# A routed expert stage with its slot table read in one load, a later first split of w_in, and gate steps placed ahead of the w2 splits

## The reference

```python
attn_out = _attn_ref(x, state)                 # two cross reads: x (8,8,512,64), state (8,8,32,64)
x = attn_out.transpose(0, 2, 1, 3).reshape(B * S, H * D)     # 4352 rows of 512

# routed experts: E = 8, F = 1024
logits = xn @ en.T / tau                       # xn, en: rows divided by their norm
expert_idx = np.argmax(logits, axis=1)
gate_w = softmax(logits)[expert_idx]
for e in range(E):
    h = np.maximum(x[mask] @ w1[e], 0.0)
    out[mask] = gate_w[mask, None] * (h @ w2[e])

# dense block: d_ff = 2048
r = np.maximum(x @ w_in, 0.0)
return (s * (r * r) + b) @ w_out
```

## Time and profile before

| | us |
|---|---|
| median of 3 runs | 1513.04 (1512.64 to 1514.85) |
| profiled execution | 1512.6 |
| its span, first to last instruction | 1510.9 |
| PE busy | 1361.9 (90%) |
| DVE busy | 656.1 (43%) |
| ACT busy | 510.0 (34%) |
| POOL busy | 146.9 (10%) |

### The profile page before, as it was taken

The page is one execution under the profiler, slowest core; times in us unless marked ns, Lnnn a source line. Parts: engine busy times, 40 slices in busy tenths (PEclk is TensorE's granted clock), DMA queues, the critical chain, the costliest instruction groups (busy, mean ns, idle before and its releaser), DMA issues.

```text
span 1510.9 us, 22781 instructions
## 1 busy us (share of the span) xinstructions
PE 1361.9 (90%) x6875; PEld 1123.5 (74%) x6876; DVE 656.1 (43%) x1646; ACT 510.0 (34%) x977; POOL 146.9 (10%) x186
## 2 busy tenths in 40 slices
PE   5887224999999999999899999999999999999995
PEld 4655213787888888887788888888888888888884
DVE  4766512456656456555652232323223232322322
ACT  3655202345545345444332222222222222222221
POOL 1222210001111001101400010100001010000101
PEclk9988556999999999999899999999999999999998
DMA  8752212434434124314100010100101010010000
GB/s 214 144 122 64 63 16 51 151 110 162 159 115 168 43 104 164 111 43 168 42 15 29 1 56 0 56 0 14 42 0 56 0 56 0 0 56 0 28 0 28
DMA packets 81043, 100.07 MB, mean 66 GB/s; under 512 B 50152, under 2 KB 50408, under 8 KB 79984
## 3 DMA queue, kind: packets, MB, share of 16 engines
q1 hardware_dynamic: 68336, 69.59, 15.7%
q0 software_dynamic: 7200, 20.08, 4.1%
q10 hardware_dynamic: 5472, 9.96, 1.7%
HBM read 71.11 MB, written 28.64 MB: 66 GB/s over the span
## 4 chain that ended last, share of the span: by engine, by line
PE 79%; DVE 5%; issue 4%; ACT 3%; SPq 3%; DMA 2%; ACTq 2%; POOL 1%; DVEq 0%; another core or an unknown queue 0%; POOLq 0%
PE bank_a L1343 25%; PE bank_n L1362 13%; PE bank_t L1362 12%; PE bank_a L1277 10%; PE bank_n L1302 10%; DVE w_lo L963 1%; PE bank_t L1288 1%; PE bank_t L1112 1%; SPq L337 1%; SPq L384 1%; DMA x_tok<-st_rows 1%; PE bank_a L1095 1%; PE bank_n L1264 1%; ACT x_rows L555 1%; PE bank_a L1183 1%
## 5 line engine op out<-in xcount | busy, mean ns | idle before, releaser
L1047 DVE TENSOR_TENSOR sq<-rel 128x512 f32<-128x512 f32 (+1 forms) x144 | 95.5, 663 | 484.6 <-ACT rel L710 484.6
L710 ACT ACTIVATE rel<-bank_a 128x512 f32<-128x512 f32 (+1 forms) x144 | 82.8, 575 | 548.1 <-PE bank_a L1343 548.1
L1343 PE MATMUL bank_a<-y_hi,w_in_hi 128*128 128x512 f32 (+1 forms) x576 | 218.9, 380 | 4.6 <-DVE y_lo L1039 4.5
L1343 PE MATMUL bank_a<-y_hi,w_in_lo 128*128 128x512 f32 (+1 forms) x576 | 218.4, 379 | 0.0
L1343 PE MATMUL bank_a<-y_lo,w_in_hi 128*128 128x512 f32 (+1 forms) x576 | 218.3, 379 | 0.0
L1343 PEld LDWEIGHTS bank_a<-y_hi,w_in_hi 128*128 128x128 f32 x576 | 109.4, 190 | 26.2 <-DVE y_lo L1039 5.0
L1343 PEld LDWEIGHTS bank_a<-y_lo,w_in_hi 128*128 128x128 f32 x576 | 109.4, 190 | 20.6 <-issue 0.2
L1343 PEld LDWEIGHTS bank_a<-y_hi,w_in_lo 128*128 128x128 f32 x576 | 109.4, 190 | 20.1
L1302 PE MATMUL bank_n<-w_hi,hid_hi 128*128 128x512 f32 x304 | 119.1, 392 | 4.2 <-DVE hid_lo L970 4.2
L1302 PE MATMUL bank_n<-w_lo,hid_hi 128*128 128x512 f32 x304 | 119.0, 391 | 0.0
L1302 PE MATMUL bank_n<-w_hi,hid_lo 128*128 128x512 f32 x304 | 119.0, 391 | 0.0
(11 more groups left out here) (198 smaller groups left out, 2082.1 us busy)
## 6 DMA issues: line engine op xcount, KB each, us to landing
w_raw<-in_moe_w SPq DMA_DIRECT2D x16, 2048.0 KB, 9.7
moe_tok<-yg ACTq DMA_DIRECT2D x38, 256.0 KB, 2.0
x_tok<-x_rows SPq DMA_DIRECT2D x8, 1088.0 KB, 5.7
x_m<-in_x SPq DMA_DIRECT2D x8, 1024.0 KB
y_rows<-moe_tok SPq DMA_DIRECT2D x8, 1024.0 KB, 5.1
win_raw<-in_moe_w_in SPq DMA_DIRECT2D x8, 512.0 KB, 9.7
w_raw<-in_moe_w_out SPq DMA_DIRECT2D x1, 4096.0 KB, 15.1
idx_all<-slot_tab SPq DMA_DIRECT2D x43, 0.5 KB, 2.0
```

Source lines behind the costliest of these rows:

```text
L710: nc.scalar.activation(rel[:, k, 0:cols], ps_g[k][:, 0:cols], ACT.Relu).then_inc(rel_ready, 1)
L1047: nc.vector.tensor_tensor(sq[:, 0:cols], rel[:, k, 0:cols], rel[:, k, 0:cols], ALU.mult).then_inc(sq_ready, 1)
L1343: last = nc.tensor.matmul(ps_g[n % 2][:, 0:cols], w[:, wc], a[:, c, 0:cols], start=(c == 0 and w is w_in_hi and a is y_hi), stop=(c == DC ...
```

## The change

The slot table is now f32 and has room for TCAP·128 = 4608 entries per expert, 36 tiles' worth. SP reads all of it in one DMA into `slot_sb` (96 partitions, 3 pieces of 128 words); PE turns the three pieces into one PSUM bank, and DVE casts them into `idx_all`, which now has a column for every possible tile (288). A tile's column number is `slots_of`, read by POOL before each copy. SP's loads of w_in chunk 0 and of expert 1's weights follow the first gather directly, and the eight copies to `moe_id` (now f32) come after them. The ids for the scatter are loaded as f32 and cast by POOL. On ACT and DVE the split of w_in chunk 0 moves behind the hidden split of tile 0. In DVE's loop the gate steps of tile g+3 move ahead of the w2 splits.

```diff
+    TCAP = (NTOK + P - 1) // P + 2
+    TQ = E * TCAP // 3
-    CAP = NTOK
-    ZCOLS = (E * CAP + 8 * P) // P
+    CAP = TCAP * P
+    ZCOLS = E * CAP // P
...
+        slot_sb = sb(am, "slot_sb", [TQ, 3, P], f32)
+        sb(am, "hole", [P, 1408], f32)
+        idx_all = sb(am, "idx_all", [P, E * TCAP], i32)
...
-            def load_idx(g, done):
-                src = slot_tab[0:P, :] if g == 0 else slot_tab[ds(slots_of(sp, g), P), :]
-                sp.dma_start(idx_all[:, g:g + 1], src).then_inc(done, 16)
+            def copy_ids():
+                for e in range(E):
...
             sp.wait_ge(slots_written, 16 * (TPB + 1) * B)
-            with nc.allow_non_contiguous_dma(reason="one word per row"):
-                load_idx(0, idx_first)
-                sp.wait_ge(tab_ready, 1)
-                for g in range(1, NEAR):
-                    load_idx(g, idx_next)
-                sp.wait_ge(gathered, 16)
-                for g in range(NEAR, NSLOT):
-                    load_idx(g, idx_loaded)
+            sp.dma_start(slot_sb[:], slot_tab.rearrange("(k t q) o -> t k (q o)", k=3, q=P)).then_inc(slot_loaded, 16)
+            sp.wait_ge(tab_ready, 1)
+            sp.wait_ge(gathered, 16)
             load_win(0)
-            for e in range(E):
...
             for e in range(1, E):
                 sp.wait_ge(w1_ready, WS * e)
                 sp.dma_start(w_raw[:, 0:WCOLS], w1[e].rearrange("(c p) n -> p c n", p=P)).then_inc(w1_loaded, 16)
...
                 load_win(e)
                 sp.wait_ge(w2_ready, WS * e)
                 sp.dma_start(w_raw[:, WCOLS:2 * WCOLS], w2[e].rearrange("(c p) n -> p c n", p=P)).then_inc(w2_loaded, 16)
+                if e == 1:
+                    copy_ids()
...
-                nc.gpsimd.tensor_copy(g_idx[:], idx_all[:, ds(g, 1)]).then_inc(idx_turn, 1)
+                nc.gpsimd.tensor_copy(g_idx[:], idx_all[:, ds(0 if starts(g) else slots_of(pool, g), 1)]).then_inc(idx_turn, 1)
...
             def scatter(u, n):
                 pool.wait_ge(oid_loaded, 16 * u + 16)
+                pool.sem_inc(scatter_turn, 1)
+                nc.gpsimd.tensor_copy(out_id[:, 0:n], out_idf[:, 0:n]).then_inc(oid_ready, 1)
+                pool.wait_ge(oid_ready, u + 1)
...
             act.wait_ge(tab_ready, 1)
-            win_hi(0)
             gate_square(1)
...
             hidden_hi(0)
+            win_hi(0)
...
-            tab_step(nc.vector.tensor_scalar(t_in, t_in, float(P), None, ALU.mult))
-            tab_step(nc.vector.scalar_tensor_tensor(o_slot, o_e, float(CAP), t_in, ALU.mult, ALU.add))
-            tab_step(nc.vector.tensor_tensor(o_row, t_row, t_in, ALU.add))
+            tab_step(nc.vector.scalar_tensor_tensor(o_slot, o_e, float(TCAP), t_in, ALU.mult, ALU.add))
+            tab_step(nc.vector.scalar_tensor_tensor(o_row, t_in, float(P), t_row, ALU.mult, ALU.add))
...
-            for k in range(2 * WS):
+            for k in range(WS):
+                split_lo(k)
+            dve.wait_ge(slot_tr, 1)
+            nc.vector.tensor_copy(idx_all[:], bank_r[:, E:E + 3 * TQ]).then_inc(idx_ready, 1)
+            for k in range(WS, 2 * WS):
                 split_lo(k)
...
             gate_scale(0)
-            win_lo(0)
             gate_final(0)
...
             hidden_lo(0)
+            win_lo(0)
...
             def tile(g):
...
                 hidden_lo(g + 1)
+                gate_scale(g + 3)
                 next_w2(g)
-                gate_scale(g + 3)
...
             nc.tensor.matmul(bank_r[:, 0:E], ones_b[:], pre5[:, TPB + 1, :], start=True, stop=True).then_inc(tot_mm, 1)
+            pe.wait_ge(slot_loaded, 16)
+            pe.wait_ge(tab_link, 1)
+            for k in range(3):
+                last = nc.tensor.transpose(bank_r[:, E + k * TQ:E + (k + 1) * TQ], slot_sb[:, k, :], ident[0:TQ, 0:TQ])
+            last.then_inc(slot_tr, 1)
```

More of the change, by code:

```diff
@@ L49, in attention_moe_ffn @@
     RW = PAIRS * GW
-    CAP = NTOK
-    ZCOLS = (E * CAP + 8 * P) // P
+    CAP = TCAP * P
+    ZCOLS = E * CAP // P
     WOS = FC2 * D // SLOT
-    assert PAIRS == 4 and HEAD == 2 and TPB == 4 and WS == 4 and HB == 2
+    assert E * TCAP == 3 * TQ and TQ <= P and PAIRS == 4 and HEAD == 2 and TPB == 4 and WS == 4 and HB == 2
     def row_col(j):
@@ L58, in attention_moe_ffn @@
     x_tok = nc.dram_tensor("x_tok", [NTOK, RW], f32, kind="Internal").ap()
-    slot_tab = nc.dram_tensor("slot_tab", [ZCOLS * P, 1], i32, kind="Internal").ap()
+    slot_tab = nc.dram_tensor("slot_tab", [ZCOLS * P, 1], f32, kind="Internal").ap()
     moe_tok = nc.dram_tensor("moe_tok", [NTOK + 4 * P, D], f32, kind="Internal").ap()
-    moe_id = nc.dram_tensor("moe_id", [NTOK + CAP, 1], i32, kind="Internal").ap()
+    moe_id = nc.dram_tensor("moe_id", [NTOK + CAP, 1], f32, kind="Internal").ap()
     top = ExitStack()
@@ L87, in attention_moe_ffn @@
         out_id = sb(top, "out_id", [P, TROWS], i32)
+        out_idf = sb(top, "out_idf", [P, TROWS], f32)
         lg = sb(top, "lg", [P, E], f32)
@@ L92, in attention_moe_ffn @@
         gi = sb(top, "gi", [P, 2], i32)
-        used = sum(-(-n // 32) * 32 for n in (4 * P, 4 * P, 2 * P, 2 * P, 4 * PAIRS * E, 4 * RW, 4 * (4 * NSLOT + 1 + E), 4 * NSLOT, 4 * NSLOT,
-                                              4, 4, 4, 4 * TROWS, 4 * E, 4 * E, 4 * E, 32, 8))
+        used = sum(-(-n // 32) * 32 for n in (4 * P, 4 * P, 2 * P, 2 * P, 4 * PAIRS * E, 4 * RW, 4 * (4 * NSLOT + 1 + E), 4 * NSLOT,
+                                              4, 4, 4, 4 * TROWS, 4 * TROWS, 4 * E, 4 * E, 4 * E, 32, 8))
         sb(top, "line_pad", [P, (128 - used % 128) // 4], f32)
@@ L136, in attention_moe_ffn @@
         inv_tau = sb(am, "inv_tau", [P, 1], f32)
-        zero_i = sb(am, "zero_i", [P, ZCOLS], i32)
+        zero_f = sb(am, "zero_f", [P, ZCOLS], f32)
         m1 = sb(am, "m1", [P, TPB * H], f32)
@@ L154, in attention_moe_ffn @@
         order_m = sb(am, "order_m", [P, TPB + 1, E], f32)
-        ids = sb(am, "ids", [P, B, TPB + 1], i32)
+        ids = sb(am, "ids", [P, B, TPB + 1], f32)
         slot_f = sb(am, "slot_f", [P, NSLOT], f32)
@@ L268, in attention_moe_ffn @@
         wout_ready = sem("wout_ready")
-        idx_loaded = sem("idx_loaded")
-        idx_first = sem("idx_first")
-        idx_next = sem("idx_next")
+        slot_loaded = sem("slot_loaded")
+        slot_tr = sem("slot_tr")
+        idx_ready = sem("idx_ready")
+        oid_ready = sem("oid_ready")
         idx_turn = sem("idx_turn")
@@ L336, in slots_of @@
         def slots_of(eng, g):
-            return eng.value_load(tile_tab[0:1, ds(2 * NSLOT + g, 1)], min_val=0, max_val=ZCOLS * P - P)
+            return eng.value_load(tile_tab[0:1, ds(2 * NSLOT + g, 1)], min_val=0, max_val=E * TCAP - 1)
         def rows_of(eng, g):
@@ L366, in _ @@
             sp.wait_ge(tab_zero, 1)
-            sp.dma_start(slot_tab.rearrange("(p n) o -> p (n o)", p=P), zero_i[:]).then_inc(tab_cleared, 16)
+            sp.dma_start(slot_tab.rearrange("(p n) o -> p (n o)", p=P), zero_f[:]).then_inc(tab_cleared, 16)
             for bb in range(B):
@@ L453, in _ @@
                                     pattern=[[-1, P]], channel_multiplier=1).then_inc(const_ready, 1)
-            nc.gpsimd.memset(zero_i[:], 0).then_inc(tab_zero, 1)
+            nc.gpsimd.memset(zero_f[:], 0).then_inc(tab_zero, 1)
             nc.gpsimd.memset(ones_b[:], 1.0).then_inc(const_ready, 1)
@@ L464, in _ @@
                                     pattern=[[-2 * P, TPB + 1], [0, E]], channel_multiplier=-1).then_inc(const_ready, 1)
-            nc.gpsimd.iota(ids[:, :, 0:TPB], pattern=[[ROWS, B], [1, TPB]], base=0, channel_multiplier=TPB).then_inc(tab_zero, 1)
-            nc.gpsimd.iota(ids[:, :, TPB:TPB + 1], pattern=[[ROWS, B], [0, 1]], base=S, channel_multiplier=1).then_inc(tab_zero, 1)
+            nc.gpsimd.iota(ids[:, :, 0:TPB], pattern=[[ROWS, B], [1, TPB]], base=0, channel_multiplier=TPB,
+                           allow_small_or_imprecise_dtypes=True).then_inc(tab_zero, 1)
+            nc.gpsimd.iota(ids[:, :, TPB:TPB + 1], pattern=[[ROWS, B], [0, 1]], base=S, channel_multiplier=1,
+                           allow_small_or_imprecise_dtypes=True).then_inc(tab_zero, 1)
             nc.gpsimd.iota(slot_f[:], pattern=[[1, NSLOT]], base=0, channel_multiplier=0,
@@ L494, in _ @@
             pool.wait_ge(st_stored, 16 * B)
-            pool.wait_ge(idx_first, 16)
+            pool.wait_ge(idx_ready, 1)
             gather(0)
-            pool.wait_ge(idx_next, 16 * (NEAR - 1))
+            pool.wait_ge(tab_ready, 1)
             gather(1)
```

15 lines of the change are left out of this document (6 added, 9 removed).

## The result

The changed kernel took 1504.66 us in the median of 17 runs (1499.46 to 1510.82), the kernel before 1513.49 us beside it (17 runs, 1510.29 to 1515.88): a ratio of 0.9945, 95% interval 0.9932 to 0.9957. It is faster, by 0.5%, where 1.5% was forecast, and its time lies outside the forecast's range of 1476 to 1498. The profiled execution was the fastest of the 17: 1499.5 us, a span of 1497.8. Against the profiled execution before (1512.6) that is −13.1 us, and the traces are compared at that pair first.

| stretch | forecast, us | in the traces, us |
|---|---|---|
| head, to the third tile's turn | −36.5 | −39.7 (278.39 to 238.65) |
| third tile's turn to the 38th's, with the seven changes of expert | +13.4 | +26.5 |
| all else (from the 38th tile's turn to the end: 792.0 before, 792.1 after) | 0 | about 0 |
| sum | −23.1 | −13.1 |

What follows compares the result with a forecast made beforehand. TensorE, busy 90% of the span, was taken to bound the kernel, its head held by SyncE's issue rate through ACT's order. 1512.6 − 33.4 − 0.8 − 2.3 + 13.4 = 1489.5 us, range 1476 to 1498.

Steps and rivals of the forecast that it cites:

- The views and the bound: Whole kernel: TensorE bounds it, busy 90% of the span; its dwarfing wait is 37.1 us before the hidden block's first turn.
- Part 1: Slot table's path to the first gather: grows by 4.2 us, POOL's copy waiting until the w2 splits end.
- rival (a): First gather: POOL's copy slips in after the first w2 split, saving 3.4 us, 1486.1 us; within the forecast's 0.73.
- the row of 1.70 us: Before's first POOL copy, 0.18 us elsewhere, took 1.70 beside the w2 splits; read as held past a split boundary.
- the loop's row: POOL's copy in the loop: 0.78 us from 345.46, over with the first split of a group, so held by one split.
- Part 2: Head, early loads and later split: −33.4 us for the wait, −0.8 for the clock, −2.3 for the first store.
- Part 3: Seven changes of expert: gate steps ahead delay the w2 splits, TensorE stalls 3.7 us each, net +13.4 us.
- (b): Changes of expert: gate steps lie in idle time, only their wait goes, −12.7 us instead of +13.4, 1463.4 us; chance 0.07.
- (d): Changes of expert: gate steps wait for a late gather, holding up the w2 splits; slower, some 1528 us; chance 0.03.
- (c): Head: early w1 load slows second and third gathers, third tile 4 to 8 us later, 1493.5 to 1497.5; chance 0.13.
- (e): Head: ACT's next wait, for the second gather, is as long as the old one; only +13.4 left, 1526; chance 0.02.

## Why the prediction was wrong

**The views and the bound** were right: the one wait of 37 us is gone, and with it 39.7 us of the head. Some luck is in that number: the writes to the table ended 2.6 us later behind their last issue than before (8.8 for 6.2), which the forecast left out, and after's last write happened to go out 2.8 us earlier.

**Part 1** was 2.7 us too dear. The load (2.7 for 2.4), the three transposes (0.74 for 0.8) and the cast (0.46 for 0.45) came as priced. POOL's copy did not wait for four splits: it began at 192.34, the splits at 192.10, and it ended at 193.36. A single one of these splits takes 1.22 us, so the first ended at 193.32. That is rival (a): the row of 1.70 us that I followed was the wrong neighbour, the loop's row the right one. The Trainium skill (SBUF — State Buffer, Who interferes with whom) says that a VectorE instruction with two SBUF inputs contends with a GpSimd instruction that reads SBUF, and that the first to issue holds the shared ports for the whole instruction; it speaks of one instruction, not of a row of them. The 1.02 us of after's copy, which ended 0.04 us after the first split, agree with it, and all nine traces with the single load show 1.02. What held the copy of the earlier trace rows for 1.70 us past a boundary no run explains. Of the 3.4 us that rival (a) gives, 0.7 went again, since the first gather's issue took 1.71 us for 1.01: it landed at 197.7 for 196.2 before, +1.5 and not +4.2.

**Part 2** held, with its terms. The second gather took 6.6 us beside the w1 load (6.9 forecast) and was hidden under the first up-projection; the third landed 3.4 us after its issue; the second up-projection started 2.45 us earlier than forecast, which is Part 1's gain, and took 6.8 us for 8.11 (−1.3; −0.8 was forecast). TensorE's wait of 2.31 us behind the first store is gone. A wait was avoided here that I had not priced: that the later split keeps w2's load from the third gather, worth 2.8 us in one pair of traces.

**Part 3 is the step that failed.** Its mechanism was right: the splits start 5.95 us behind the start of the low hidden split, for 2.18 before, so 3.8 late (3.9 forecast), TensorE waits 3.7 us at the first change, 25.1 in seven (3.7 each forecast), and the low split of x is no longer late. But the term was mis-sized, +13.4 for a measured +26.5, because it ended with the wait. Behind the pause the granted clock falls, and the 24 matmuls take 7.1 us and more for 5.5; over seven changes the down-projections take 12.5 us longer than with the gate steps back (51.8 for 39.3 us). The trace of before had a row for this: in Part 2 I charged the up-projection 1.6 us for a pause of 1.9. I applied that row at the head, where the pause was old, and not at the changes, where the change makes seven new ones, each longer. Seven times 1.6 would have given +24.6, and 1500.7 us in all.

That row alone was no sure price, though. The same trace has a pause of 2.31 us at 272.84 behind which the clock stayed at 1.00 and the 24 matmuls took 5.7 us. And the pause of 1.9 us before the last down-projection is in all thirteen traces: in three the matmuls behind it took 7.3 us, with a lower clock, in the ten others 5.7. After's:

```profile
709.40:715.20 5.80, 5.72 (x24) 4.42 (x24) 1.00 0.00 0
```

The pauses of 3.3 to 3.7 us are another matter: behind 27 of the 28 in the four traces that have them the clock fell. From before's trace alone a term between 0 and 1.6 us per change was to be had, not its upper end.

**The rivals.** Between (b), that the gate steps lie in idle time, and (d), that the changes cost more, the direction was (d)'s, with another mechanism: nothing waited for a gather. (c) and (e) didn't occur.

**The level.** Of the 15.2 us between 1489.5 and 1504.66, 10 lie in the traces (13.1 of Part 3, less 3.2 of the head). The other 5.2 lie between after's profiled execution, the fastest of its 17, and their median. After's runs spread over 11.4 us, before's over 5.6. The trace of its repetition (1508.19 us) shows where: the table load goes out at 195.48, 7.2 us later, with 10.3 us behind the last write, the first turn 6.5 us later, and the changes 1.5 us longer. Of the 7.2 us, 1.5 lie behind the last write (10.3 for 8.8 us), in a table of the same room, and 5.8 ahead of it, where the last write went out at 185.19 for 179.41; why is unexplained. My range took one execution's head as the typical one.

**The kernel to keep** has the head of the change and the old order of the gate steps: ratios of 0.9773 and 0.9799 to before in two sets, 1.7 and 1.5% below the changed kernel's. Room for 39 tiles with it gave 1475.40 us, the lowest of all medians, but in the set in which the kernel before was low as well.

## What to carry to other kernels

When an edit makes TensorE wait in a stage where it had been working without a break, price the wait and then look at what every pause of that kind in the trace did to the matmuls behind it, not at one; here the clock behind the pause doubled the cost. When two edits attack one wait, ask what each does with the other in place. Here one edit removed the cause, 43 small loads ahead of a big one in SyncE's queue, and with it in place the edit that steps around the wait brought nothing that could be measured. And a trace is one execution: a stage whose length rests on many small indirect writes moves by several us between executions, so the range needs that much in addition.

## What the runs showed of the hardware

- After pauses of TensorE of 3.3 to 3.7 us the granted clock fell from 2.4 GHz to 1.2 GHz for part of the down-projection at six of seven changes (0.76 over the 24 matmuls of the first), and at all seven in each of the three other traces with these pauses. After a pause of 1.9 us it fell in three traces of thirteen. With 3.29 us of useless matmuls in the pause it stayed at 1.00. The useless work gives back 12 us of the stage; not pausing gives back 26.5.
- The indirect writes of single words reached the waiting queue 6.2 to 7.8, 8.8 to 10.4 and 13.6 to 14.2 us after the last one's issue with room for 34, 36 and 39 tiles in each part of the table. The writes were the same in number (40 indirect DMAs) and size.
- An indirect gather of 128 rows took 4.1 us from issue to the copy behind it, and 8.6 us when 2.5 MB of weight loads were issued 2 us ahead of it. In the trace of before, the fifth gather, issued at 265.84 behind 4.5 MB of loads (260.5 to 261.7), landed 7.5 us after its issue.
